# Splitting the last eight pieces of the MLP's weights one or two steps later

## The reference, cut to what matters

```
attn_out = softmax(q) @ (softmax over tokens(k)^T @ v)            # 8 heads of 64
x  = attn_out as [8, 576, 512]
xn = (x - mean) / sqrt(var + 1e-6) * g_ln
x  = x + relu(xn @ w_ch1) @ w_ch2                                  # 512 -> 2048 -> 512
out = sum over the best 2 of 4 gated heads of causal attention(x, wq, wk, wv) @ wo
```

## Time and profile before

| | |
|---|---|
| median of three runs | 1230.61 us (1229.38 to 1231.84) |
| profiled execution, its own time | 1228.85 us |
| its span in the trace | 1226.7 us |
| around the span | 2.15 us |
| PE busy | 1199.0 us, 98% of the span |
| DVE, ACT, POOL busy | 668.6, 390.7, 219.2 us |
| mean granted clock of TensorE | 0.997 |

### The profile page before, as it was taken

The page is one execution under the profiler, slowest core; times in us unless marked ns, Lnnn a source line. Parts: engine busy times, 40 slices in busy tenths (PEclk is TensorE's granted clock), DMA queues, the critical chain, the costliest instruction groups (busy, mean ns, idle before and its releaser), DMA issues.

```text
span 1226.7 us, 19131 instructions
## 1 busy us (share of the span) xinstructions
PE 1199.0 (98%) x7010; PEld 998.3 (81%) x7010; DVE 668.6 (55%) x1701; ACT 390.7 (32%) x887; POOL 219.2 (18%) x244
## 2 busy tenths in 40 slices
PE   8999999999999999999999999999998999999998
PEld 7878888888888888888888888888887888878875
DVE  6775465366365365366356332321358777776762
ACT  4652131131131121121221211112254554555455
POOL 3541000000000000000000000002136565455322
PEclk9999999999999999999999999999999999999999
DMA  8831640450460370280270140150058787887762
GB/s 186 203 107 41 133 67 14 126 84 6 112 108 5 82 138 5 74 146 2 76 142 5 39 102 2 35 128 27 12 159 215 194 233 210 254 236 194 191 177 78
DMA packets 346314, 133.39 MB, mean 109 GB/s; under 512 B 242544, under 2 KB 330608, under 8 KB 346224
## 3 DMA queue, kind: packets, MB, share of 16 engines
q1 hardware_dynamic: 345696, 132.18, 44.8%
q10 hardware_dynamic: 528, 0.00, 0.0%
HBM read 72.49 MB, written 42.86 MB: 94 GB/s over the span
## 4 chain that ended last, share of the span: by engine, by line
PE 84%; DVE 5%; SPq 3%; ACT 3%; DMA 3%; issue 1%; POOL 1%; DVEq 0%; ACTq 0%; POOLq 0%
PE hb L1583 30%; PE yb L1671 30%; PE sc L1583 12%; PE ob L1829 4%; PE pa L1600 3%; SPq L727 1%; PE pa L1591 1%; PE sc L1795 1%; DMA pt<-turned 1%; PE tb L1795 1%; ACT prob L1094 1%; SPq L577 1%; DMA ksb<-in_k_dram 0%; DVE prob L1520 0%; DVE px L1502 0%
## 5 line engine op out<-in xcount | busy, mean ns | idle before, releaser
L1362 DVE SCALAR_TENSOR_TENSOR hid_lo<-hb,hid_hi 128x512 fp32r<-128x512 f32 x144 | 99.6, 692 | 388.3 <-ACT hid_hi L972 388.3
L972 ACT ACTIVATE hid_hi<-hb 128x512 fp32r<-128x512 f32 x144 | 85.9, 597 | 609.8 <-PE hb L1583 609.8
L1671 PE MATMUL yb<-hid_hi,w_hi 128*128 128x512 f32 x576 | 227.0, 394 | 2.0 <-DVE hid_lo L1362 2.0
L1583 PE MATMUL hb<-xn_hi,w_hi 128*128 128x512 f32 (+1 forms) x580 | 228.1, 393 | 0.7 <-DVE xn_lo L1421 0.7
L1583 PE MATMUL hb<-xn_lo,w_hi 128*128 128x512 f32 (+1 forms) x580 | 225.1, 388 | 0.0
L1583 PE MATMUL hb<-xn_hi,w_lo 128*128 128x512 f32 (+1 forms) x580 | 225.0, 388 | 0.0
L1671 PE MATMUL yb<-hid_hi,w_lo 128*128 128x512 f32 x576 | 224.9, 390 | 0.0
L1671 PE MATMUL yb<-hid_lo,w_hi 128*128 128x512 f32 x576 | 224.8, 390 | 0.0
L1583 PEld LDWEIGHTS hb<-xn_hi,w_hi 128*128 128x128 f32 x580 | 108.9, 188 | 26.3 <-issue 2.9
L1671 PEld LDWEIGHTS yb<-hid_hi,w_hi 128*128 128x128 f32 x576 | 108.4, 188 | 24.7 <-issue 2.4
L1583 PEld LDWEIGHTS hb<-xn_hi,w_lo 128*128 128x128 f32 x580 | 108.9, 188 | 22.8
(11 more groups left out here) (223 smaller groups left out, 1792.6 us busy)
## 6 DMA issues: line engine op xcount, KB each, us to landing
qx<-in_q_dram SPq DMA_DIRECT2D x32, 288.0 KB, 5.2
ksb<-in_k_dram SPq DMA_DIRECT2D x8, 1024.0 KB, 5.8
vsb<-in_v_dram SPq DMA_DIRECT2D x32, 256.0 KB, 4.9
stage<-in_moe_w_ch_dram SPq DMA_DIRECT2D x16, 512.0 KB, 4.1
xn_lo<-ksb SPq DMA_DIRECT2D x128, 64.0 KB, 2.0
y_scratch<-ysb SPq DMA_DIRECT2D x32, 256.0 KB, 2.9
ysb<-xsb SPq DMA_DIRECT2D x128, 64.0 KB, 2.1
out_dram<-osb SPq DMA_DIRECT2D x32, 256.0 KB, 4.4
```

The source lines that it names most:

```text
L972: act.activation(HID[f % 2][0][:], hb[f % 2][:], ACT.Relu).then_inc(sems["hhi_a"], 1)
L1362: dve.scalar_tensor_tensor(out=lo[:], in0=hb[f % 2][:], scalar=0.0, in1=plain(hi[:]), op0=ALU.max, op1=ALU.subtract).then_inc(sems["hlo_v" ...
L1583: ins = pe.matmul(dst, l, r, start=(n == 0), stop=(n == len(terms) - 1))
L1671: ins = pe.matmul(yb[j][:], l, r, start=(f == 0 and m == 0 and not first), stop=(f == FT - 1 and m == 2), skip_group_check=True)
```

## The change

One line, the table of the steps at which ACT splits the pieces, is different. Pieces 4 to 7 stay at steps 0 and 1. Pieces 8 and 9 go from step 3 to 4, pieces 10 and 11 from 5 to 7, pieces 12 and 13 from 7 to 9, pieces 14 and 15 from 9 to 11.

```diff
-        PIECES_AT = {0: [4, 5], 1: [6, 7], 3: [8, 9], 5: [10, 11], 7: [12, 13], 9: [14, 15]}
+        PIECES_AT = {0: [4, 5], 1: [6, 7], 4: [8, 9], 7: [10, 11], 9: [12, 13], 11: [14, 15]}
```

## The result

The changed kernel took 1227.93 us, median of 12 runs (1225.71 to 1228.70), against 1230.31 us for the kernel before beside it (median of 12 runs, 1228.10 to 1233.18). The ratio is 0.9972 with a 95% interval of 0.9962 to 0.9982, so 0.28% faster. Forecast were 1227.7 us and 2.94 us of gain; measured, the two medians differ by 2.4 us and the ratio stands for 3.4. The profiled execution took 1225.71 us, its span 1223.6 us, against 1226.7 before.

What follows compares the result with a forecast made beforehand. PE's chain bounds the kernel, with X0's start set by DVE's kvn. Copies -3.86 us and exponentials +0.92 us sum to -2.94 us, from 1230.61 to 1227.7 us; range 1225.7 to 1230.6 us.

Steps and rivals of the forecast that it cites:

- The limit behind the limit: At X0, first chunk: DVE's kvn sets the start, 5.26 us after hid_lo(6) starts; the lower clock costs almost nothing.
- The copies: DVE's four copies of line 1316, first chunk: 0.85 us instead of 4.71 without POOL's low parts beside them, -3.86 us.
- Pieces 8 and 9: Move from step 3 to 4: hid_hi(5) 0.92 us late; one blocked keys' subtraction is covered by 1.1 us.
- The margin of 0.30 us: At the keys' subtractions: DVE's fourth starts 0.30 us ahead of POOL's first low part.
- two blocks: Rival at the keys' subtractions: POOL blocks the fourth and fifth, gain only 1.4 us, 1229.2 us; chance 0.16.
- X0: Its start after the MLP's step 7: at 84.69 us instead of 87.63, with PE waiting about 0.8 us.
- Pieces 12 to 15: Moves to steps 9 and 11: cost nothing, bounds 0 and 1 us.
- The clock rival: Lower clock in front of X0 or at 926 to 934 us: 1.7 us per fall, two give 1231.1 us; chance 0.06.
- nothing is given back later: From X0 to the MLP's end, PE's matmuls follow each other at 2.72 us per twelve, so the 2.94 us stays.

Runs made afterwards that it cites:

- The control: The kernel before, unchanged, run again under another name; 1230.55 us, ratio 0.9997.
- the filled kernel: The kernel before plus 16 small unread matmuls in front of mlp2(6), filling PE's wait; ratio 0.9979, run again 0.9998.
- e1: The change, but with pieces 8 and 9 kept at step 3; 1227.48 us, ratio 0.9970.
- e4: The kernel before with pieces 12 to 15 moved to steps 9 and 11, and POOL's low part of piece 10 waiting for the queries' subtraction; 1227.27 us, 0.9964.
- e6: The change, but with the gains of piece 8 applied at step 3 so POOL can start its low part earlier; 1228.19 us, ratio 0.9960.
- e2: The kernel before with only pieces 8 and 9 moved, from step 3 to 4; 1231.10 us, ratio 1.0005.
- e3: The kernel before with only pieces 12 to 15 moved, to steps 9 and 11; 1230.84 us, ratio 0.9994.
- g4: Second run of the change with pieces 8 and 9 kept at step 3; 1226.09 us, ratio 0.9969.
- g3: The change run again, unaltered; 1225.86 us, ratio 0.9955.

## Why the prediction was right

**The limit behind the limit.** The prediction said that DVE's kvn sets X0, and that PE's wait and the lower clock in front of it were two losses over a stretch that was lost anyway. The control, where X0 waits for line 1173 at full clock, and the filled kernel show it. Whoever had added the wait (2.04 us) and the slow matmuls (1.7 us) would have forecast a gain of 3.75 us from the change instead of the 3.15 that came. e1 and e4 show where that limit lies: there kvn ends just as PE gets to X0, which comes 3.76 and 3.77 us earlier, and no wait is left.

**The copies.** Forecast: from 4.71 to 0.85 us, at 74.3. Measured: 0.85 us, at 73.92. e4 shows that moving the low parts away is enough.

**Pieces 8 and 9.** Forecast: hid_hi(5) 0.92 us late, one subtraction of five shut out, covered by ACT. Measured, from hid_hi(3): 0.70 us late (13.61 against 12.91), the five subtractions 5.30 us (about 5.4 forecast), and no idle time between ACT's exponentials. From the first of them to hid_hi(5) it is 2.62 us, not 2.94: the distance of 0.59 us that I multiplied was too long for five that follow each other without a wait. With the terms as measured, -3.86 + 0.70 = -3.16, which is the 3.15 of the traces. This term was 0.2 us too large, the only one of the sum that was off.

**The margin of 0.30 us** to the case of two blocks held in both executions of the change (5.30 and 5.29 us for the five). e6 shows what lay behind it: 1.14 us. e2, in which pieces 8 and 9 stand at step 4 too, has 5.29 us.

**X0.** Forecast 84.69 with PE idle for 0.8 us, measured 84.34 with 0.59.

**Pieces 12 to 15** cost nothing that the runs can tell, as forecast; e3 has no change in time, and PE waits nowhere at steps 8 to 15 of the change.

**The clock rival** did not come at X0: the new idle stretch of 0.59 us was followed by a clock of 1.00. In the third layer the clock fell at 931 us, as it had at 934 before:

```profile
931.00:934.50 3.50, 3.50 (x17) 2.62 (x17) 3.26 (x15) 1.51 (x7) 0.71 (x2) 0.52 0.86 220
```

But there was one more fall in the change, at 1207.5 us, where the profile of before has none. The prediction's rival looked for a fall in front of X0 or at 926 to 934 us and not there. The windows, and PE's rows of the same 20 matmuls, of the change:

```profile
1207.50:1211.00 3.50, 3.50 (x20) 1.85 (x16) 0.33 (x2) 0.39 (x3) 1.09 (x2) 0.52 0.00 0
```
```profile
1207.13 3.96 PE L1829 MATMUL ob<-pt,v 128*64 128x320 f32 x20
```

And before:

```profile
1210.50:1214.00 3.50, 2.63 (x24) 1.51 (x22) 0.41 (x4) 1.83 (x6) 1.31 (x3) 1.00 0.00 0
```
```profile
1211.89 2.28 PE L1829 MATMUL ob<-pt,v 128*64 128x320 f32 x20
```

It cost 3.96 - 2.28 = 1.68 us, the price that the prediction had set for a fall. That it doesn't show in the span has another reason. From X0 to PE's first wait of that place (line 1807, at 1205.28 us, and at 1210.05 before) it is 1120.94 us instead of 1122.42, 1.5 us less, since PE's waits in front of line 1829 in the third layer came to 5.2 us (3.9 for DMAs and 1.3 for "issue") instead of 6.9 (4.5 and 2.4). These waits scatter between executions of one kernel (4.0 us in the control), so the forecast span of 1223.8 us, met within 0.2, and "nothing is given back later" owe something to luck. Of the six profiles in which the low parts of pieces 10 and 11 miss the copies, five have this late fall (all but g4); of the other six only e2 has it. Whether the change brings it about is not shown.

**What stays open.** The two timings of the change, 0.28% and 0.45%, are both above what X0's shift of 3.15 us, or 0.26%, would give; the first has it well within its interval, the second has not (0.33% at least). What makes the second larger is not shown. The record points to the clock elsewhere in the span: the mean granted clock was 0.998 over the six executions of g3 and 0.996 over the twelve of the control, where one fall of 3.5 us to 0.52 takes 0.0014 off the mean. The forecast that the gain would lie just beyond what can be told from no change was right for the first.

## What to carry to other kernels

When an engine on the critical path waits and then runs at a lower clock, don't add the two: look for who else would have made it wait at the end of that stretch. Before moving work off a busy engine, look at whom the work's follow-up on another engine meets; here it was not ACT's 3.65 us that counted but the 4.7 us of GpSimd work that it sets off. When a span agrees with a forecast, look whether a loss and a gain elsewhere cancel in it. A cheap way to test such a meeting is one more wait on the follow-up, without moving anything else.

## What the runs showed of the hardware

Where they held each other up, DVE and POOL took turns, instruction by instruction. A pair of low parts of 2.37 us each held up two DVE instructions where both met some: two copies before (4.71 us for the four instead of 0.85), a copy and a maximum in e2, two subtractions in e6 (7.51 us for the five instead of 3.08). In the change the first low part held up one subtraction (5.30 us for the five), and the second waited for that one and found none behind it. The length of the DVE instruction mattered little: two copies that take 0.2 us undisturbed lost 3.86 us together, two subtractions of 0.6 us lost 4.43.

Not every DVE instruction was held up. In e4 the low parts run from 79.17 to 83.94 us beside hid_lo(6) and the four transposes of the queries, which take 0.69 and 2.75 us there, as they do in the change (0.69 and 2.75 us), where POOL is idle. So e4's place for the low parts cost nothing up to X0.

The clock fell behind some of PE's waits and not behind others. In front of mlp2(6), the waits of 2.04 us (before), 2.42 us (e3) and 3.08 us (e2) were followed by a clock of 0.52 to 0.53, the one of 1.79 us in the control was not. Whether it was the length of the wait that made the difference, or something else, is not shown.
